# Head 9 of a fused attention and two-MLP kernel: its probabilities transposed by DMA as two fp16 planes instead of by TensorE

## The reference

```python
scores = scale * (q @ k.T)                         # per head, 576 x 576
x = log1p(|i - j|) / log1p(max(i, 1))
bias = relu(x * w1 + b1) @ w2                      # one 576 x 576 table per head
attn = exp(scores + bias - max); attn /= (attn.sum(-1) + 1e-9)
o = attn @ v                                       # 2304 tokens x 512
g = s * relu(o @ w_in) ** 2 + b;   x = g @ w_out   # 512 -> 2048 -> 512
h = x @ w2_in;   y = (h - tanh(h)) @ w2_out        # 512 -> 2048 -> 512
```

## Time and profile before

| | us |
|---|---|
| median of 3 runs (1090.86 to 1090.99) | 1090.95 |
| the profiled execution | 1089.92 |
| its span | 1088.1 |
| TensorE matmul busy | 1050.2 (97%) |
| TensorE weight load busy | 912.5 (84%) |
| ScalarE busy | 728.4 (67%) |
| GpSimd busy | 690.6 (63%) |
| VectorE busy | 625.1 (57%) |

### The profile page before, as it was taken

The page is one execution under the profiler, slowest core; times in us unless marked ns, Lnnn a source line. Parts: engine busy times, 40 slices in busy tenths (PEclk is TensorE's granted clock), DMA queues, the critical chain, the costliest instruction groups (busy, mean ns, idle before and its releaser), DMA issues.

```text
span 1088.1 us, 16872 instructions
## 1 busy us (share of the span) xinstructions
PE 1050.2 (97%) x5685; PEld 912.5 (84%) x5685; DVE 625.1 (57%) x1128; ACT 728.4 (67%) x1469; POOL 690.6 (63%) x656
## 2 busy tenths in 40 slices
PE   6679999999999999999999999999999999999998
PEld 2168889888888888888888888888888888999998
DVE  7968877655775475567747755761450451440640
ACT  8978888767878587777758766873562553552652
POOL 1056666687778778868876887766454455455553
PEclk9999999999999999999999999999999999999999
DMA  5788867799889788998996799764333333333331
GB/s 191 252 251 261 269 196 175 198 253 230 211 214 259 205 210 237 238 212 196 255 268 164 184 274 245 186 145 134 106 116 98 99 115 125 119 121 101 96 122 64
DMA packets 185338, 201.19 MB, mean 185 GB/s; under 512 B 125811, under 2 KB 129829, under 8 KB 185253
## 3 DMA queue, kind: packets, MB, share of 16 engines
q1 hardware_dynamic: 185108, 200.04, 67.2%
q10 hardware_dynamic: 144, 0.07, 0.1%
HBM read 155.23 MB, written 15.64 MB: 157 GB/s over the span
## 4 chain that ended last, share of the span: by engine, by line
PE 70%; ACT 14%; issue 7%; DVE 6%; DMA 2%; POOL 1%; SPq 0%; DVEq 0%; ACTq 0%; POOLq 0%
PE ps_f L919 19%; PE ps_f L921 19%; PE ps_f L920 19%; ACT x_raw L345 2%; PE ps_o L555 2%; DVE g_buf L979 2%; PE ps_s L594 2%; ACT planes L642 2%; ACT gh L932 2%; DVE g_buf L982 2%; PE ps_s L595 1%; PE ps_o L558 1%; PE ps_o L570 1%; ACT ps_t L654 1%; ACT gh L936 1%
## 5 line engine op out<-in xcount | busy, mean ns | idle before, releaser
L876 POOL TENSOR_TENSOR wl<-w_raw,wh 128x512 fp32r<-128x512 f32 x318 | 418.3, 1320 | 255.9 <-ACT wh L869 254.8
L919 PE MATMUL ps_f<-gh,wh 128*128 128x464 f32 (+1 forms) x640 | 242.7, 379 | 2.3 <-DVE g_buf L979 1.7
L919 PE MATMUL ps_f<-xh,wh 128*128 128x464 f32 (+1 forms) x640 | 240.5, 376 | 0.6 <-DVE ptl L748 0.6
L921 PE MATMUL ps_f<-xh,wl 128*128 128x464 f32 (+1 forms) x640 | 237.4, 371 | 0.0
L920 PE MATMUL ps_f<-gl,wh 128*128 128x464 f32 (+1 forms) x640 | 237.4, 371 | 0.0
L921 PE MATMUL ps_f<-gh,wl 128*128 128x464 f32 (+1 forms) x640 | 237.2, 371 | 0.0
L920 PE MATMUL ps_f<-xl,wh 128*128 128x464 f32 (+1 forms) x640 | 237.1, 370 | 0.0
L869 ACT ACTIVATE wh<-w_raw 128x512 fp32r<-128x512 f32 x318 | 196.6, 623 | 48.4 <-PE ps_f L921 48.2
L919 PEld LDWEIGHTS ps_f<-gh,wh 128*128 128x128 f32 x640 | 120.8, 189 | 16.0 <-DVE g_buf L979 2.8
L919 PEld LDWEIGHTS ps_f<-xh,wh 128*128 128x128 f32 x640 | 120.5, 188 | 13.4 <-DVE ptl L748 0.8
L921 PEld LDWEIGHTS ps_f<-xh,wl 128*128 128x128 f32 x640 | 120.1, 188 | 13.4
(11 more groups left out here) (126 smaller groups left out, 1694.8 us busy)
## 6 DMA issues: line engine op xcount, KB each, us to landing
w_raw<-in_w_out SPq DMA_DIRECT2D x80, 512.0 KB, 3.6
w_raw<-in_w_in SPq DMA_DIRECT2D x79, 512.0 KB, 3.5
bias_t<-bias_flat SPq DMA_DIRECT2D x128, 288.0 KB, 4.0
bias_flat<-stage SPq DMA_DIRECT2D x36, 295.5 KB, 2.2
k_raw<-in_kt SPq DMA_DIRECT2D x32, 288.0 KB, 4.1
q_raw<-in_qt SPq DMA_DIRECT2D x32, 288.0 KB, 3.6
v_raw<-in_vt SPq DMA_DIRECT2D x22, 288.0 KB, 3.2
bias_t<-bias_flat SPq DMA_DIRECT2D x32, 144.0 KB, 4.3
```

The source lines that it names most:

```text
L876: pool.tensor_tensor(wl[:, b % RING, :, :], raw_block(b), wh[:, b % RING, :, :].bitcast(F32), ALU.subtract).then_inc(w_lo_done, 1)
L919: pe.matmul(acc, hi, rhs_h[:, k0 + kk, 0:T], start=(first and kk == 0), stop=False)
L921: mm = pe.matmul(acc, lo, rhs_h[:, k0 + kk, 0:T], start=False, stop=(last and kk == 3))
```

## The change

`TURNED` goes from 10 to 9: head 9 is now turned by DMA as two planes, divided before the product with the values, and head 8 is the last one that TensorE turns. Heads are paired for the late division, and head 8 has no partner now, so it is divided alone (64 partitions, in step 52, where the pair 8 and 9 was divided in step 56). Head 9 takes over `p_even` and `p_odd`, and with them one more wait (on VectorE's own earlier work); head 10 leaves its scores in PSUM. The third home of the planes comes into use from step 56 where it was step 61.

```diff
-TURNED = 10
+TURNED = 9
...
             if 2 * pair < TURNED:
                 eng.wait_ge(x_done, pair + 1)
-            else:
+            if 2 * pair + 1 >= TURNED:
                 eng.wait_ge(o_done, 2 * pair + 2)
...
             if t == 1 and n >= 2 and n % 2 == 1 and n - 2 < TURNED:
-                pool_scale(pool, n - 2)
+                pool_scale(pool, (n - 3, n - 2))
                 if n == H + 1:
                     pool_split(pool, KD - 1)
+            if t == 2 and n == TURNED + 1 and TURNED % 2:
+                pool_scale(pool, (n - 2,))
...
-        def pool_scale(pool, h):
-
-            for m in (h - 1, h):
+        def pool_scale(pool, heads):
+
+            for m in heads:
                 pool.wait_ge(inv_loaded[m % 2], (m // 2 + 1) * DMA)
-            pool.wait_ge(o_done, h + 1)
-            x = x_slice(h, slice(0, P))
-            pool.tensor_tensor(x, x, inv_b[:], ALU.mult).then_inc(x_done, 1)
+            pool.wait_ge(o_done, heads[-1] + 1)
+            rows = slice(0, len(heads) * D)
+            x = x_slice(heads[0], rows)
+            pool.tensor_tensor(x, x, inv_b[rows, :], ALU.mult).then_inc(x_done, 1)
...
                 if t == 0 and n < TURNED:
                     need(dve, pt_done, (n - 1) * NT)
+                if n == TURNED:
+                    need(dve, p_lo_done, t - 1)
```

## The result

The changed kernel takes **1094.84 us** (median of 8 runs, 1092.48 to 1095.61) against 1090.7 (8 runs, 1089.61 to 1091.34) for the kernel before on the same chip: ratio 1.0034, 95% interval 1.0025 to 1.0042. By the ratio that is 3.7 us slower (the two medians are 4.1 us apart), past the 0.2% that the forecast took as what a measurement can tell, and above the upper end of the forecast range.

A forecast was written before the change was run, and what follows sets the result against it. TensorE bounds the kernel from the first MLP matmul on; just before, TensorE, VectorE and ScalarE hold each other up. Terms -2.8 + 4.5 - 0.5 = +1.2, counted +1.1, gave 1092.0 us, range 1089.2 to 1094.3.

The forecast's parts named there:

- The chain, +4.5: Steps 46 to 48: added plane work on VectorE and ScalarE delays the first MLP matmul from 151.88 to 156.4, +4.5 us.
- the hops: Steps 46 to 48: sum to reciprocal and upper to lower plane cannot overlap with anything in the written order.
- Step 48: Upper plane of strip 47 could start at 153.6 but waits until 154.0 for strip 45's home to be free.
- TensorE's work, -2.8: Steps 50 to 54: five strips of head 9's transposes go, 2.7 us, plus 0.1 for the small transpose of inverses.
- Later stalls, -0.5: Later in unit 0: TensorE stalls of 0.53 and 0.39 go, -0.9; a longer second-stage wait adds 0.45.
- unit 0 would look like unit 1: First block of unit 0's second stage would wait 0.70 as in unit 1, not 0.25: +0.45 us.
- same: Whole kernel: a time between 1088.8 and 1093.1 us, not distinguishable from no change; chance 0.67.
- rival 3: TensorE, between 147 and 156 us: its clock falls; three us at half clock lose 1.5, giving 1093.5; chance 0.06.
- rival 4: Unit 0's first blocks: crowding on ScalarE, VectorE and GpSimd makes TensorE wait 2 us in all, 1094; chance 0.06.
- Homes (2): Step 48: waiting for one of two plane homes makes the start up to 6.8 late, +3.5, 1094.5; chance 0.12.
- Late planes (5): Step 52: head 9's planes arrive by DMA too late for their product, +5, 1097; chance 0.02.
- Hidden work (1): Before the MLP: added vector work fills VectorE's gaps, only +1.9 paid, 1089.0 to 1089.5; chance 0.17.

The follow-up runs named there:

- the second trace: The changed kernel run and traced once more, unedited, against the kernel before: 1095.39 us, ratio 1.0041.
- the last two variants: Changed kernel with VectorE's reciprocal right behind the minimum and lower plane last, without and with repeated scores: 1090.98 and 1090.85 us, ratios 1.0002 and 1.0004 to before.
- the last variant without repeats: Changed kernel with VectorE's reciprocal right behind the minimum and the lower plane last, no scores repeated: 1090.98 us, ratio 1.0002 to the kernel before.

## Why the prediction was wrong

**The chain, +4.5: right in size.** Counted from minimum 45, the forecast had the next minima at 2.86, 6.56 and 9.36 and the first MLP matmul at 12.06. The trace has 2.91, 6.70, 9.65 and 11.92. It rested on the minimum waiting behind the reciprocal, and that does not bind: with the minimum first, `x_raw` came no sooner (5.83 against 5.84). What binds is that head 8's lower part stands behind a lower plane that waits for the upper one: moving the lower plane behind the lower part and `x_raw` took 1.5 to 2.1 us off the chain of the first trace. That the hops "can't overlap with anything in the written order" was true, and the written order was the thing to question. The close hit is in part luck. Step 48 had 0.4 us of waiting for a home (153.6 to 154.0) that did not happen, and the lower plane was priced at 0.82 from the earlier trace rows, whose scores lie in PSUM; those of head 9 lie in SBUF, and the second one took 1.17.

**TensorE's work, -2.8: right.** With the clock at 1.00 the first stage without its stall is 48.16 against 51.20 before, -3.04.

**Later stalls, -0.5: right in sign, small miss.** Both stalls went (the next stage is 0.70 shorter, of 0.92 forecast). The stall at the second stage grew to 0.95 to 0.97, not 0.70. The run with transposes left out shows that the stall also grows (0.25 to 1.35) when only transposes go: it is the transposes' gain being given back, and the forecast's reason, that unit 0 would look like unit 1, was not the cause.

**The sum without the clock.** The repeated scores give it: distance 267.11 against 265.65, +1.46, where the terms above (4.5 - 2.35 - 0.92) give +1.23. Its timed ratio of 1.0015 would have been within the forecast's "same".

**The failed step is the clock.** The sum took 1.00 throughout, and rival 3 had a chance of 0.06. Its "against" was "the idle pieces are short". They were: 1.05 and 1.25 us in the two longest before the fall. Its "for" was right, that TensorE would do about half its time nothing. The share of work could have been had from the forecast: 7.42 us in 8.30, stretched by 4.5, is 58%, and the trace has 3.50 of 6 us. But no row of the kernel before says whether such a share brings a fall; the only fall in those rows followed a wait of 4.29. The forecast priced a fall at 1.5 us, from three us at half clock. It lasted over 6 us in the first trace and cost 1.2 us on the distance, since more than half of it lay before the first MLP matmul, where VectorE set the pace. In the second trace there were two, and they cost 1.7 us, or 2.6 with the long lower plane that the lateness brought about. In the timed runs, keeping TensorE busy in that stretch gave back 2.9 us.

The Trainium skill (TensorE: Matmul & The Clock Gate, section A second HAM failure mode: psum-queue depth-cycling) tells of a kernel whose TensorE idled briefly but often, and whose clock went back and forth between the two levels. By that, short waits can bring a fall; the trace of the changed kernel agrees, with waits of 1.05 and 1.25 us. That they need not, another run shows: with the reciprocal right behind the minimum the waits were 1.02 and 1.41, and the clock stayed at 1.00. The prediction leaned on the sentence of Part 1 and then argued it away with the length of single pieces.

**A signature that misled.** By the forecast, over 50 us from the first MLP matmul to the second stage would mean crowding, and so 50.39 would have been read as rival 4. The rows say otherwise: TensorE is busy 49.43 of 50.32 us with one stall, at a clock of 0.97. Such a length alone does not tell a slow matmul from a waiting one.

**The other rivals.** Homes (2): excluded, the third upper plane waited for its reciprocal. Late planes (5) and crowding (4): no such wait of TensorE between 203 and 226, and only the one of 0.95 in the 50.32 us of the first stage. Hidden work (1): no, though with the lower plane last part of it hides.

**Open.** The forecast's 1092.0 and the measured 1094.84 are 2.8 apart. The clock, with what it brought about, makes 1.2 to 2.6 of it by the traces and 2.9 by the medians with and without the repeats, so the size is known only roughly. Another 0.35 lies outside the span: time less span is 1.75 to 1.92 in every timed run of the kernel before in the three sets, and 2.08 to 2.27 in every run of the changed kernel and its variants. It comes with the change, and why stays open. It is one reason why the last two variants, 0.5 to 0.8 shorter than before on the distance, are only level in time; but the medians of their spans are level too (1088.8 and 1088.7 against 1088.6), so the timed runs do not confirm the shorter distance. The mean clocks say that the fall came in most runs of the changed kernel; where it lay in each, only the two traces tell.

## What to carry to other kernels

When an edit slows the engine that feeds TensorE, price TensorE's clock too, and look at its busy time in the stretch that gets longer, not only at its single waits. Where it is open whether the clock or a wait costs the time, a run with repeated harmless matmuls in the waits separates the wait's cost from the clock's. An instruction that waits for another engine belongs behind the work of its own engine that somebody else waits for; and time taken off the busiest engine is kept only as far as the next engine's result is ready.

## What the runs showed that I had not expected

- The clock fell to 0.50 with no single wait over 1.25 us in the stretch before, at 3.50 busy of 6 us. With repeated scores in the same steps (5.20 of 6) it stayed at 1.00.
- More work made the kernel faster: repeated scores on TensorE, 1095.39 to 1092.52.
- VectorE's lower plane, 0.82 us elsewhere, took up to 1.50 with both planes further back and up to 1.87 in the last variant without repeats, and the rows tie this to GpSimd. The twelve traces have 60 lower planes whose scores lie in SBUF (`p_even`, `p_odd`). 40 of them took longer than 0.82, and each of these began while a GpSimd instruction was running and ended 0.60 to 0.63 after it. With the scores in PSUM, none of the 105 in the trace of before took over 0.82. It works the other way too: GpSimd's L212 took 2.02 where the plane began 0.08 or less before it, and 1.40 where it was first.
- The part of a fall that lies before the first MLP matmul can cost nothing: from 154 to 158 the changed kernel ran at 0.64 and 0.50 and its chain was still 11.92, against 12.03 at full clock. In its second trace the fall came at 152, and there it made VectorE 0.5 late and the chain 13.21.
